# GpSimd without arithmetic in a bilinear layer, with combined weights made earlier and kept in DRAM

## What is computed

```python
def _moe2_ref(x, w_a, w_b, w_out):        # x (2304, 512), w_a and w_b (512, 1536), w_out (1536, 512)
    a = x @ w_a
    b = x @ w_b
    return (a * b @ w_out)
```

## Time and profile before

| | |
|---|---|
| median of 3 runs | 880.26 us (878.06 to 881.4) |
| profiled execution, its own time | 880.36 us |
| its span, first to last instruction | 878.2 us |
| mean granted TensorE clock | 0.965 |
| busy: TensorE, VectorE, ScalarE, GpSimd | 808.1, 573.0, 330.3, 284.6 us |
| first and last product of the bilinear layer start | 377.8, 853.7 us |

### The profile page before, as it was taken

The page is one execution under the profiler, slowest core; times in us unless marked ns, Lnnn a source line. Parts: engine busy times, 40 slices in busy tenths (PEclk is TensorE's granted clock), DMA queues, the critical chain, the costliest instruction groups (busy, mean ns, idle before and its releaser), DMA issues.

```text
span 878.2 us, 14879 instructions
## 1 busy us (share of the span) xinstructions
PE 808.1 (92%) x5345; PEld 745.8 (85%) x5346; DVE 573.0 (65%) x944; ACT 330.3 (38%) x565; POOL 284.6 (32%) x211
## 2 busy tenths in 40 slices
PE   8999989999999999979699888798889987999996
PEld 6888859999999999978589888687888887889885
DVE  5577785546446445668776777767776768776772
ACT  4565625435434444333324332223333323223230
POOL 2000030110111011245753446616453365333342
PEclk9999969999999999989999999989999999999999
DMA  9887626724743764344121123411121213212201
GB/s 213 203 236 204 189 70 207 244 82 184 254 133 137 238 201 139 98 117 131 49 70 51 48 73 121 139 48 54 49 72 48 70 51 120 72 51 71 72 1 72
DMA packets 129683, 102.76 MB, mean 117 GB/s; under 512 B 63485, under 2 KB 107551, under 8 KB 129631
## 3 DMA queue, kind: packets, MB, share of 16 engines
q1 hardware_dynamic: 125311, 91.12, 34.0%
q0 software_dynamic: 4176, 10.92, 4.3%
q10 hardware_dynamic: 144, 0.04, 0.0%
HBM read 87.04 MB, written 15.04 MB: 116 GB/s over the span
## 4 chain that ended last, share of the span: by engine, by line
PE 78%; DVE 11%; issue 8%; ACT 2%; POOL 1%; another core or an unknown queue 0%; POOLq 0%; DVEq 0%; ACTq 0%
PE pz L1862 25%; PE po L1889 14%; PE py L1805 12%; PE pu L1794 9%; PE pu L1776 3%; DVE g L1441 3%; PE pscore L1575 2%; PE pout L1624 2%; PE pu L1784 2%; PE pout L1599 2%; DVE g L1469 1%; PE pq L1563 1%; PE px_tok L1586 1%; PE pstate L1611 1%; PE px L1753 1%
## 5 line engine op out<-in xcount | busy, mean ns | idle before, releaser
L741 POOL TENSOR_TENSOR w_lo<-w_land,w_hi 128x768 fp32r<-128x768 f32 x72 | 153.1, 2139 | 238.9 <-DVE w_land L1389 156.6
L1862 PE MATMUL pz<-x_hi,w_hi 128*128 128x384 f32 x504 | 181.0, 359 | 53.3 <-DVE g L1441 38.4
L1862 PE MATMUL pz<-x_hi,w_lo 128*128 128x384 f32 x504 | 177.2, 352 | 0.0
L1862 PE MATMUL pz<-x_lo,w_hi 128*128 128x384 f32 x504 | 177.2, 352 | 0.0
L1862 PEld LDWEIGHTS pz<-x_hi,w_hi 128*128 128x128 f32 x504 | 100.9, 200 | 66.0 <-POOL w_lo L741 31.9
L948 ACT CAST w_hi<-w_land 128x768 fp32r<-128x768 f32 x72 | 67.8, 944 | 104.4 <-DVE w_land L1389 100.3
L1862 PEld LDWEIGHTS pz<-x_lo,w_hi 128*128 128x128 f32 x504 | 100.8, 200 | 0.6
L1862 PEld LDWEIGHTS pz<-x_hi,w_lo 128*128 128x128 f32 x504 | 100.7, 200 | 0.0
L1469 DVE TENSOR_TENSOR g<-g,a_sb 128x384 f32<-128x384 f32 x54 | 83.3, 1542 | 1.9
L1889 PE MATMUL po<-wo_hi,g_hi 128*128 128x512 f32 x216 | 84.2, 390 | 0.0
L1889 PE MATMUL po<-wo_hi,g_lo 128*128 128x512 f32 x216 | 84.2, 390 | 0.0
(11 more groups left out here) (245 smaller groups left out, 1571.9 us busy)
## 6 DMA issues: line engine op xcount, KB each, us to landing
land<-in_moe_w_dram SPq DMA_DIRECT2D x64, 512.0 KB, 8.8
w_land<-in_moe_w_a_dram SPq DMA_DIRECT2D x72, 128.0 KB, 2.3
w_land<-in_moe_w_b_dram SPq DMA_DIRECT2D x72, 128.0 KB, 2.3
wo_land<-in_moe_w_out_dram SPq DMA_DIRECT2D x18, 512.0 KB, 3.5
y_columns<-y_out SPq DMA_DIRECT2D x8, 672.0 KB, 6.0
q_in<-in_q_dram SPq DMA_DIRECT2D x16, 256.0 KB, 3.5
k_in<-in_k_dram SPq DMA_DIRECT2D x16, 256.0 KB, 4.1
v_in<-in_v_dram SPq DMA_DIRECT2D x16, 256.0 KB, 4.3
```

The source lines that it names most:

```text
L741: nc.gpsimd.tensor_tensor(w2_lo[unit % 3][:, at, :, :], w2_land[unit % 3][:, at, :, :], w2_hi[unit % 3][:, at, :, :], ALU.subtract).then_i ...
L1862: ins = nc.tensor.matmul(pz[n % 2][:, 0:T], w, m, start=(k in FRESH and j == 0 and i == 0), stop=(j == DH2 - 1 and i == 2), skip_group_che ...
```

## The change

Seven of the twelve weight units (0 to 6) are now made beside the experts, one in the first window of each of the experts 0 to 6: SP loads the raw quarters behind the next expert's weights, VectorE combines, ScalarE and VectorE split, and SP stores high and low parts, 1.8 MB, to a DRAM tensor `w2_dram`. The five others (`RAW`, units 7 to 11) are made in the first pass as before, but with the low parts on VectorE, and are stored too. Everything else, units 0 to 6 in the first pass and all units in the later ones, is loaded ready from `w2_dram`. GpSimd's subtractions and combinations go to VectorE; x low parts are made in the steps that `X_IN_STEP` names. GpSimd keeps the gathers and scatters. The first output weights are loaded ahead of unit 2. The diff, cut to its core; the rest renames semaphores and moves `combine_w2` and `combine_x2` to forms that take a buffer or a pair.

```diff
+    RAW = range(E - 1, 2 * NQ)
...
+    w2_dram = nc.dram_tensor("bilinear_weights", (2 * NQ, 2, P, NPR * DH2 * P), f32, kind="Internal").ap()
...
+        PARTS = (slice(A12, A21), slice(0, A12))
+        X_IN_STEP = {2: range(4), NQ - 1: range(4, NPR)}
...
-            def load_w2(unit):
-                w = (w_a, w_b)[unit % 2].rearrange("(h j p) (q i f) -> p h q i j f", h=2, j=DH2, p=P, q=NQ, i=2)
+            def load_raw(w, block, n, landed):
+                quarters = w.rearrange("(h j p) (g f) -> p h j g f", h=2, j=DH2, p=P, f=P)
                 for half, at in ((0, A11), (1, A12)):
                     for i in range(2):
-                        sp.dma_start(w2_land[unit % 3][:, at + i, :, :],
-                                     w[:, half, unit // 2 % NQ, i, :, :]).then_inc(w2_in[unit % 3], 16)
+                        sp.dma_start(w2_land[n][:, at + i, :, :].unsqueeze(2),
+                                     quarters[:, half, :, bass.ds(block + i, 1), :]).then_inc(landed, 16)
+            def store_w2(unit, n, stored):
+                for part, m in ((0, w2_hi[n][:]), (1, w2_lo[n][:, 0:NPR, :, :])):
+                    sp.dma_start(w2_dram[bass.ds(unit, 1), part, :, :].rearrange("o p n -> p (o n)"),
+                                 m.rearrange("p k j f -> p (k j f)").bitcast(f32)).then_inc(stored, 16)
+            def load_w2(unit):
+                n, kept = unit % 3, unit % (2 * NQ)
+                if split_in_place(unit):
+                    load_raw((w_a, w_b)[unit % 2], unit // 2 * 2, n, raw_in[unit - RAW[0]])
+                    return
+                for part, m in ((0, w2_hi[n][:]), (1, w2_lo[n][:, 0:NPR, :, :])):
+                    sp.dma_start(m.rearrange("p k j f -> p (k j f)").bitcast(f32), w2_dram[kept, part, :, :]).then_inc(w2_in[n], 16)
...
+                    sp.wait_ge(stage_stored, e * 32 + 32)
+                    sp.sem_inc(alone_sp, 1)
+                    load_raw((w_a, w_b)[s], e - s, 0, stage_in)
...
+                if first:
+                    sp.wait_ge(stage_lo_done, e * 2 + 2)
+                    sp.sem_inc(alone_sp, 1)
+                    store_w2(e, 0, stage_stored)
...
+                sp.wait_ge(stage_stored, 32 * E)
+                load_w2(0)
                 load_w2(1)
...
+            load_wo(0)
             load_w2(2)
-            load_wo(0)
             load_wo(1)
...
+            def refill(unit):
+                if unit < 2 * NIT:
+                    sp.wait_ge(multiplied, (unit - 2) * NPR)
+                    if split_in_place(unit - 3):
+                        sp.wait_ge(raw_stored[unit - 3 - RAW[0]], 32)
+                    load_w2(unit)
...
+                for unit in (2 * step + 1, 2 * step + 2):
+                    if split_in_place(unit):
+                        sp.wait_ge(raw_lo_done, 2 * (unit - RAW[0]) + 2)
+                        store_w2(unit, unit % 3, raw_stored[unit - RAW[0]])
+                refill(2 * step + 4)
...
-            def low_w2(unit, part):
-                if part == 0:
-                    pool.wait_ge(w2_made, unit + 1)
-                pool.wait_ge(w2_hi_done, 2 * unit + part + 1)
-                at = slice(A12, A21) if part == 0 else slice(0, A12)
-                nc.gpsimd.tensor_tensor(w2_lo[unit % 3][:, at, :, :], w2_land[unit % 3][:, at, :, :], w2_hi[unit % 3][:, at, :, :],
-                                        ALU.subtract).then_inc(w2_lo_done, 1)
...
-            for step in range(NIT):
-                pair, q = step // NQ, step % NQ
-                if step < NIT - 1:
-                    for part in range(2):
-                        low_w2(2 * step + 2, part)
-                if step == 0:
-                    pool.wait_ge(wo_hi_done, 1)
-                    nc.gpsimd.tensor_tensor(wo_lo[0][:], wo_land[0][:], wo_hi[0][:], ALU.subtract).then_inc(wo_lo_pool, 1)
-                if q == 0 and pair > 0:
-                    scatter(pair - 1)
-                if step < NIT - 1:
-                    for part in range(2):
-                        low_w2(2 * step + 3, part)
-                if pair < NP - 1:
-                    if q == 1:
-                        combine_x2(pair + 1)
-                    for k in range(2 * q - 4, min(2 * q - 2, NPR)):
-                        if k >= 0:
-                            low_x2(pair + 1, k)
-                if q == NQ - 1:
-                    gather_gates(pair)
-            scatter(NP - 1)
+            for pair in range(NP):
+                gather_gates(pair)
+                scatter(pair)
...
+                if first:
+                    for part in range(2):
+                        if part == 0:
+                            act.wait_ge(stage_in, e * 64 + 64)
+                        else:
+                            act.wait_ge(stage_made, e + 1)
+                        nc.scalar.copy(w2_hi[0][:, PARTS[part], :, :], w2_land[0][:, PARTS[part], :, :]).then_inc(stage_hi_done, 1)
...
+            def split_high(unit):
+                i = unit - RAW[0]
+                act.wait_ge(raw_in[i], 64)
+                nc.scalar.copy(w2_hi[unit % 3][:, PARTS[0], :, :], w2_land[unit % 3][:, PARTS[0], :, :]).then_inc(raw_hi_done, 1)
+                act.wait_ge(raw_made, i + 1)
+                nc.scalar.copy(w2_hi[unit % 3][:, PARTS[1], :, :], w2_land[unit % 3][:, PARTS[1], :, :]).then_inc(raw_hi_done, 1)
...
+                if first:
+                    dve.wait_ge(stage_in, e * 64 + 64)
+                    combine_w2(0, stage_step, e * 3, stage_made)
+                    dve.wait_ge(stage_made, e + 1)
+                    for part in range(2):
+                        dve.wait_ge(stage_hi_done, e * 2 + (part + 1))
+                        low_w2(0, part).then_inc(stage_lo_done, 1)
...
+            def split_low(unit):
+                i = unit - RAW[0]
+                dve.wait_ge(raw_in[i], 64)
+                combine_w2(unit % 3, raw_step, 3 * i, raw_made)
+                dve.wait_ge(raw_made, i + 1)
+                for part in range(2):
+                    dve.wait_ge(raw_hi_done, 2 * i + part + 1)
+                    low_w2(unit % 3, part).then_inc(raw_lo_done, 1)
...
+                    for unit in (2 * step + 1, 2 * step + 2):
+                        if split_in_place(unit):
+                            split_low(unit)
                     low_wo(step)
+                    if pair < NP - 1:
+                        if q == 1:
+                            combine_x2(pair + 1)
+                        for k in X_IN_STEP.get(q, ()):
+                            low_x2(pair + 1, k)
...
-                    if k < 2:
-                        pe.wait_ge(w2_lo_done, 2 * unit + k + 1)
+                    if split_in_place(unit):
+                        if k < 2:
+                            pe.wait_ge(raw_lo_done, 2 * (unit - RAW[0]) + k + 1)
+                    elif k == 0:
+                        pe.wait_ge(w2_in[unit % 3], 32 * ready_units(unit))
                     if kind == 0 and step % NQ == 0:
-                        if step > 0:
-                            pe.wait_ge(x2_lo_pool, step // NQ * NPR - 4 + k + 1)
-                        elif k < DC:
-                            pe.wait_ge(x2_lo_dve, k + 1)
-                        else:
-                            pe.wait_ge(x2_lo_pool, k - DC + 1)
+                        pe.wait_ge(x2_lo_done, step // NQ * NPR + k + 1)
```

More of the change, by code:

```diff
@@ L474, in g_of, with split_in_place, ready_units @@
             return g_last if step == NIT - 1 else g_first
+        def split_in_place(unit):
+            return unit in RAW
+        def ready_units(unit):
+            return sum(1 for u in range(unit % 3, unit + 1, 3) if not split_in_place(u))
+        PARTS = (slice(A12, A21), slice(0, A12))
+        X_IN_STEP = {2: range(4), NQ - 1: range(4, NPR)}
         MADE_X = {T1: 1, T3: 2, T2: 3, T4: 4}
@@ L653, in _ @@
                 if step % NQ == NQ - 1 and pair < NP:
-                    sp.wait_ge(x2_made_pool, 4 * (pair - 1))
+                    sp.wait_ge(x2_made, 4 * pair)
                     load_x2(pair)
@@ L1042, in _ @@
                     break
-                if step == 1:
-                    high_w2(3, 0)
-                    high_w2(3, 1)
-                high_w2(2 * step + 2, 0)
-                high_w2(2 * step + 2, 1)
+                for unit in (2 * step + 1, 2 * step + 2):
+                    if split_in_place(unit):
+                        split_high(unit)
                 high_wo(step)
                 if pair < NP - 1:
-                    for k in range(2 * q - 4, min(2 * q - 2, NPR)):
-                        if k >= 0:
-                            high_x2(pair + 1, k)
+                    for k in X_IN_STEP.get(q, ()):
+                        high_x2(pair + 1, k)
                 if q == 0:
@@ L1349, in _, with combine_w2, low_w2 @@
                 turn_window(0, d, py[d])
+            def combine_w2(n, step, done, made):
+                w = w2_land[n]
```

(29 more changed lines are left out.)

133 lines of the change are left out of this document (38 added, 95 removed).

## The result

The changed kernel takes 816.06 us (812.83 to 816.8), the one before 880.41 beside it: a ratio of 0.927, 95% interval 0.924 to 0.930. The forecast was 808 us, range 795 to 834. The profiled execution took 816.8 us for a span of 815.1.

The account below looks back on a forecast made before the run. TensorE bounds the kernel, losing idle time and clock in the bilinear layer to VectorE and GpSimd taking turns. 376.3 + 4 + 412 + 1 + 1 + 3 + 8.8 = 806, plus 2: 808 us, range 795 to 834.

Parts of the forecast that it names:

- Start, 376.3: Handover to the bilinear layer: TensorE starts at 376.3 instead of 377.8, x combinations no longer delaying an x turn by 1.5 us.
- the experts, 4: Seven expert windows: added transfers delay weights and the x turn; charged 4 us, bounds 0 and 14.
- The rival that the experts pay: Expert windows: store and raw load delay weights, 2 to 4 us per window, total 818 to 832; chance 0.20.
- 412 for 18 steps: Bilinear layer: 18 unhindered steps of 22.9 us, 412 against 491.6, once GpSimd's arithmetic no longer takes turns with VectorE.
- The rival that turns were not the cause: Bilinear layer: `times_a` stays near 1.6 us, only the w_lo wait and some half clock go; 835 to 845, chance 0.08.
- Two of the prediction's signs: Signs of being right: TensorE idle before pz under 10 us, and its clock at 1.0 in all slices after the first third.
- Unit 2 late, 1: Layer start: unit 2 loads only once the last window has left its place; charged 1 us (0 to 3).
- raw steps, 1: First pass, steps 3 and 4 with two raw units each: VectorE's work just fits; bound 0 to 1 us per step, 1 charged.
- Small things, 3: Transfers in the layer: nothing charged except 3 us for two gate steps and first use of stores.
- Tail, 8.8: End of the kernel: 8.8 us from 869.4 to the end, taken over from the kernel before.
- ends near 194.2: Expert window: VectorE's y_out copies, behind inserted unit work, end near 194.2, leaving 1.3 us spare, so TensorE sees nothing.
- The prediction's "only": Port rule: exclusive only for VectorE operations with two SBUF inputs against a GpSimd operation that reads SBUF.

Follow-up runs that it names:

- no_staging: The changed kernel without the seven units made beside the experts; all twelve are loaded raw and made in the first pass: 839.1 us.
- pool_dummy_read: The changed kernel plus 80 GpSimd subtractions in the bilinear layer's steps 1 to 16, results unused: 888.1 us, ratio to the kernel before 1.010.

## Why the prediction came out as it did

The forecast was right in its mechanism: GpSimd's arithmetic stretched `times_a`, and without it the clean step takes what was forecast. The total came out 8 us short, and that closeness is in part luck: one term was 13.6 us too small, others together 4 too large. Term by term:
- **Start, 376.3, and the experts, 4.** The layer's first product starts at 377.2, so that both together measured 0.9 in excess of 376.3 and not 4. The last expert window, with the handover, takes 31.4 us in place of 32.7, near the 1.5 us of gain forecast; the experts begin 0.7 us later. Each of the seven windows ahead of it lasts 30.9 to 31.0 us in the kernel before, in the changed one and in `no_staging`. The delay was as forecast: in one window the first weight came at 205.33 and the x turn at 212.12. But TensorE lost nothing by it, busy 30.90 of 30.90 us, so the charge was too high. The rival that the experts pay has nothing behind it.
- **412 for 18 steps.** Right: 22.8 to 23.2 us wherever nothing special happens. `pool_dummy_read` shows that the turns of the two engines are enough for the whole loss, since it brings back steps of 27.0 without any wait for GpSimd. The rival that turns were not the cause falls with that, and with 558 ns of median for `times_a`. Two of the prediction's signs were missed by a little, idle time of 10.7 us before pz where it said under 10, and a clock under 1.0 around step 6.
- **Unit 2 late, 1, raw steps, 1.** Neither cost anything to speak of (steps 3 and 4 take 22.8 and 23.2). In their place stands the 0.9 us for wo in step 0, which the working had not seen: it took care of the transfer of unit 2, not of the copy of wo that stands in ScalarE's queue ahead of an eviction.
- **Small things, 3.** This is the step that failed, by its size: "except 3 us for small things (two gate steps, first use of stores)". Steps 6, 12 and 1 lost 8.3, 7.0 and 1.3 us, 16.6 in all. The part-by-part said that GpSimd's indirect transfers "wait for nothing earlier than before", and left it there. But the change itself put them in a new place: with the arithmetic gone from GpSimd's program, the gathers of a pair stand right behind the scatters of the pair before, twelve indirect transfers in a row, which the diff shows. In the kernel before the six gathers went out alone (541.53 to 548.8), in a step of 25.6 us.
- **Tail, 8.8.** 8.9.

377.2 + 412 + 0.9 + 16.6 + 8.9 = 815.6, the span being 815.1.

Could the trace of before have warned? Its step 6 was long too (33.8 us against 27.1), but on another path (timelines of GpSimd, VectorE and TensorE):
```profile
565.65 0.96 POOL L788 DMA_INDIRECT out_dram<-o_sb,ids_now  x1 [0.30 <-issue]
566.64 4.12 POOL L741 TENSOR_TENSOR w_lo<-w_land,w_hi 128x768 fp32r<-128x768 f32 x2
...
566.11 5.07 DVE L1469 TENSOR_TENSOR g<-g,a_sb 128x384 f32<-128x384 f32 x1
...
571.80 0.66 PE L1862 MATMUL pz<-x_hi,w_hi 128*128 128x384 f32 x1 [4.30 <-DVE g L1441]
```
GpSimd's six scatters held up two of its subtractions, these met `times_a`, and TensorE stood 4.3 us; 1.8 more it waited for an eviction of ScalarE behind output evictions. So that excess says nothing of what twelve transfers in a row cost. When a sum takes the clean step 18 times, the steps that aren't clean in the trace of before, and those whose order the change alters, must be looked at one by one.

Three numbers of the prediction don't follow from its own terms. Its range "799 (no charges) to 816" ends at 821 if its bounds are added up (experts 14, unit 2 3, raw steps 2, small things 3). The 7.7 MB of a window are 7.8 by its terms, which leaves the 22 us as they are. The work put ahead of the y_out copies adds up to 3.95 us, which is what the trace has (189.66 to 193.60), and not to the 3 that "ends near 194.2" takes; VectorE's copies still end at 194.5, since they no longer waited for TensorE.

The rule of the Trainium skill (SBUF — State Buffer, Who interferes with whom) held in all four runs: operations of VectorE with two SBUF inputs stretch beside GpSimd's subtractions and copies, not beside its memsets, and evictions from PSUM don't stretch. The prediction's "only" is narrower than the page, which counts some copies and casts of VectorE among those that collide too; no run here tests these. The price in this kernel: five copies with one operand cost a step 0.3 us, five subtractions 4.1.

The estimate of the traffic (212 GB/s in the layer, 192 measured) was good enough. The rate taken as the queue's best, 355 GB/s, is not the ceiling: the transfers reach 401 GB/s between 385 and 400 us, above the 358 that the Trainium skill (SBUF — State Buffer, A bandwidth-pool intuition that's wrong) gives as a core's share, and with which the prediction said the 355 agreed.

## What to carry to other kernels

Before giving an idle engine work, ask which instructions of the other engines it will stretch, and whether the bottleneck's releases stand behind these in a queue. The price showed here in the duration of instructions that have no wait at all. Moving the work to where nothing waits for the stretched instruction made it free in steps 8 to 11, and not where VectorE had more to do. Transfers that GpSimd issues in a row want a look as well: here it paid to break the row and to put each group beside a stretch in which the engines hand little over. And when a forecast multiplies the clean step, list the steps that aren't clean, and what the change puts next to what.

## What the runs showed of the hardware

Indirect transfers that GpSimd issues in a row beside products delay the hand-over between TensorE, VectorE and ScalarE, although none of these has to do with the transfers. Six alone cost 0.1 to 1.8 us, twelve 5.3, eighteen 16.2 in step 1 (39.2 against 23.0), and six right behind six scatters 5.2 to 8.3. Six alone beside the output matmuls cost nothing; a longer row there was not tried. Twelve plain transfers beside products cost nothing. The cause was not found.
